# Windowed attention inside a matmul chain: scores of later chunks three slots later, VectorE's work of a round spread, first blocks on 64 keys

## The reference, cut to what matters

```python
# q, k, v: (4, 8, 576, 64); window 64
scores = q @ k.T / 8, masked to 0 <= query - key < 64
attn = softmax(scores); x = (attn @ v) as (2304, 512)
h = ((x @ w1) * (x @ w2)) @ w3 @ w_out          # w1, w2: 512x1024, w3: 1024x1024
h = h @ w_in; g = maximum(0.01 * h, h); out = g @ moe2_w_out   # w_in: 512x2048
```

## Time and profile before

| | before |
|---|---|
| median of 3 runs | 745.69 us |
| profiled execution, its own time | 744.9 us |
| its span | 743.1 us |
| PE busy | 731.5 us (98%) |
| PEld (weight loads) busy | 697.8 us (94%) |
| VectorE (DVE) busy | 533.8 us (72%) |
| ScalarE (ACT) busy | 419.1 us (56%) |
| GpSimd (POOL) busy | 96.7 us (13%) |
| granted TensorE clock | 1.00 of full speed |

### The profile page before, as it was taken

The page is one execution under the profiler, slowest core; times in us unless marked ns, Lnnn a source line. Parts: engine busy times, 40 slices in busy tenths (PEclk is TensorE's granted clock), DMA queues, the critical chain, the costliest instruction groups (busy, mean ns, idle before and its releaser), DMA issues.

```text
span 743.1 us, 13799 instructions
## 1 busy us (share of the span) xinstructions
PE 731.5 (98%) x5032; PEld 697.8 (94%) x5032; DVE 533.8 (72%) x838; ACT 419.1 (56%) x901; POOL 96.7 (13%) x122
## 2 busy tenths in 40 slices
PE   8999899999999999999999999999999999999998
PEld 7778789988889999999999999999999999999998
DVE  6988988788656868788867978658788755454552
ACT  6875587545564345566646656456678544544541
POOL 3433575403343000000000000000000000000000
PEclk9999999999999999999999999999999999999999
DMA  9884577555864289988867988988997457778773
GB/s 340 289 287 140 183 241 214 180 185 154 261 213 146 85 277 335 323 282 315 272 218 265 330 291 278 360 294 281 356 347 287 138 164 235 212 202 242 214 197 120
DMA packets 96835, 181.13 MB, mean 244 GB/s; under 512 B 7936, under 2 KB 55680, under 8 KB 96768
## 3 DMA queue, kind: packets, MB, share of 16 engines
q1 hardware_dynamic: 90032, 166.62, 68.3%
q10 hardware_dynamic: 6736, 13.63, 5.0%
HBM read 111.80 MB, written 68.42 MB: 243 GB/s over the span
## 4 chain that ended last, share of the span: by engine, by line
PE 88%; DVE 4%; DMA 3%; issue 2%; POOL 1%; ACT 1%; SPq 1%; DVEq 0%; ACTq 0%
PE acc L396 16%; PE acc L398 15%; PE acc L397 15%; PE ps_pair L398 5%; PE ps_pair L396 5%; PE ps_pair L397 5%; PE ps_more L396 4%; PE ps_more L398 4%; PE ps_more L397 3%; PE ps_values L398 3%; PE ps_values L396 3%; PE ps_values L397 3%; PE ps_values L1652 2%; PE ps_pair L1674 2%; DMA p_between<-arena 1%
## 5 line engine op out<-in xcount | busy, mean ns | idle before, releaser
L396 PE MATMUL acc<-parts,weights_a 128*128 128x384 f32 (+1 forms) x296 | 104.7, 354 | 1.7 <-DVE arena L1374 0.9
L1443 DVE TENSOR_TENSOR parts<-raw_c,parts 128x768 fp32r<-128x768 f32 x64 | 61.1, 958 | 61.5 <-ACT parts L951 61.4
L398 PE MATMUL acc<-parts,weights_a 128*128 128x384 f32 (+1 forms) x296 | 101.5, 343 | 0.0
L397 PE MATMUL acc<-parts,weights_a 128*128 128x384 f32 (+1 forms) x296 | 101.3, 342 | 0.0
L396 PE MATMUL acc<-parts,weights_b 128*128 128x384 f32 x296 | 100.8, 341 | 0.0
L398 PE MATMUL acc<-parts,weights_b 128*128 128x384 f32 x296 | 99.0, 335 | 0.0
L397 PE MATMUL acc<-parts,weights_b 128*128 128x384 f32 x296 | 99.0, 334 | 0.0
L951 ACT ACTIVATE parts<-raw_c 128x768 fp32r<-128x768 f32 x64 | 54.0, 846 | 69.0 <-DMA raw_c<-g_between 62.9
L396 PEld LDWEIGHTS acc<-parts,weights_a 128*128 128x128 f32 x296 | 55.6, 188 | 6.5 <-issue 2.4
L930 ACT ACTIVATE arena<-arena 128x384 f32<-128x384 f32 x72 | 35.9, 525 | 39.5 <-DVE arena L1316 17.5
L835 ACT ACTIVATE arena<-arena,negmax 128x128 f32<-128x128 f32 x144 | 55.8, 392 | 2.6 <-DVE negmax L1221 2.6
(11 more groups left out here) (215 smaller groups left out, 1840.0 us busy)
## 6 DMA issues: line engine op xcount, KB each, us to landing
g_between<-arena SPq DMA_DIRECT2D x75, 384.0 KB, 4.5
raw_c<-g_between SPq DMA_DIRECT2D x64, 384.0 KB, 3.5
arena<-p_between SPq DMA_DIRECT2D x42, 384.0 KB, 5.1
arena<-qk_steps SPq DMA_DIRECT2D x36, 384.0 KB, 4.1
arena<-v_steps SPq DMA_DIRECT2D x36, 256.0 KB, 3.5
p_between<-arena SPq DMA_DIRECT2D x24, 384.0 KB, 5.3
x_between<-arena ACTq DMA_DIRECT2D x21, 384.0 KB, 5.4
arena<-x_between SPq DMA_DIRECT2D x21, 384.0 KB, 5.5
```

The source lines that it names most:

```text
L396: eng.matmul(out_ap, w_hi, m_hi, start=start, stop=False, skip_group_check=resumed)
L397: eng.matmul(out_ap, w_hi, m_lo, start=False, stop=False, skip_group_check=resumed)
L398: return eng.matmul(out_ap, w_lo, m_hi, start=False, stop=stop, skip_group_check=resumed)
L1443: dve.tensor_tensor(lo, t_source(k), hi.bitcast(F32), ALU.subtract).then_inc(t_lo, 1)
```

## The change

- The scores of chunks 1 and 2 move three slots later (5, 8, ... 38 and 62, 65, ... 95), and with them everything else of a step.
- VectorE's work in a round is put elsewhere: `make_p11` from P2(1) (m = 6) to P3(0) (m = 9); `p_sums` is cut in `p_sum1`, which stays at P4(1), and `p_sums23`, which goes to the next round's P5(0) (m = -1); `make_pt4` goes to the next round's P1(0) (m = 0). `make_p22` now waits for `p_stored[0]` as well.
- At chunk ends `t1` goes from m = 5 to 7, P5's split from 6/7 to 8/9, `t2` from 9 to 10, P2's high part from 8 to 9, P6's high part from 11 to 12.
- First blocks use 64 keys: scores, mask, maximum, exponentials and normalisation have 64 columns per head pair in place of 128. Keys and values of a first block are laid in the first half, and the second half of v's rows is zero. One memset clears that half of `probs[0]` at the start, for step 0.

```diff
-        SCORES[(_c + 1) * CSTEPS + _j] = slot_of(4 * _c, 2 + 3 * _j)
+        SCORES[(_c + 1) * CSTEPS + _j] = slot_of(4 * _c, 5 + 3 * _j)
...
+def width(g):
+    return KW if g % NB else BQ
...
-XS_HI_LAST = {3: P1, 6: P5, 8: P2, 11: P6}
+XS_HI_LAST = {3: P1, 8: P5, 9: P2, 12: P6}
...
-XS_LO_LAST = {4: P1, 5: "t1", 7: P5, 9: "t2", 11: P2}
+XS_LO_LAST = {4: P1, 7: "t1", 9: P5, 10: "t2", 11: P2}
...
+            dve.memset(probs[0][:, :, BQ:KW], 0.0).then_inc(probs_zero, 1)
...
             def make_p22(r):
                 dve.wait_ge(c22_done, 2 * r + 2)
+                if r > 0:
+                    dve.wait_ge(p_stored[0], 16 * r)
...
                 if i == P2:
                     make_c11(r, s)
-                    if s == 1:
-                        make_p11(r)
...
                 if i == P3:
                     make_c12(r, s)
-                    if s == 1:
+                    if s == 0:
+                        make_p11(r)
+                    else:
                         make_p12(r)
                 if i == P4 and s == 1:
                     make_p21(r)
-                    p_sums(r)
-                    make_pt4(r)
+                    p_sum1(r)
+                    if r == AR - 1:
+                        p_sums23(r)
+                        make_pt4(r)
+                if i == P5 and s == 0 and r > 0:
+                    p_sums23(r - 1)
+                if i == P1 and s == 0 and r > 0:
+                    make_pt4(r - 1)
...
-                    last = pe.matmul(ps_scores[x, u], qk[d, g % 2, h // 2 * BQ:(h // 2 + 1) * BQ],
-                                     qk[d, g % 2, QN + u * KW:QN + (u + 1) * KW], start=True, stop=True)
+                    last = pe.matmul(ps_scores[x, u, 0:width(g)], qk[d, g % 2, h // 2 * BQ:(h // 2 + 1) * BQ],
+                                     qk[d, g % 2, QN + u * KW:QN + u * KW + width(g)], start=True, stop=True)
```

More of the change, by code:

```diff
@@ L298, in build @@
         ident_zero = sem("ident_zero")
+        probs_zero = sem("probs_zero")
         ident_made = sem("ident_made")
@@ L763, in normalize @@
                 pool.wait_ge(rsum_done, g + 1)
-                pool.tensor_tensor(probs[g % 3], probs[g % 3],
-                                   rsum[:, r * HP:(r + 1) * HP].unsqueeze(2).to_broadcast([P, HP, KW]),
+                w = width(g)
+                pool.tensor_tensor(probs[g % 3][:, :, 0:w], probs[g % 3][:, :, 0:w],
+                                   rsum[:, r * HP:(r + 1) * HP].unsqueeze(2).to_broadcast([P, HP, w]),
                                    ALU.mult).then_inc(probs_done, 1)
@@ L831, in exps @@
             def exps(g, pairs):
-                r = g % 2
+                r, w = g % 2, width(g)
                 act.wait_ge(max_done, g + 1)
                 for u in pairs:
-                    act.activation(probs[g % 3][:, u], probs[g % 3][:, u], ACT.Exp,
+                    act.activation(probs[g % 3][:, u, 0:w], probs[g % 3][:, u, 0:w], ACT.Exp,
                                    bias=negmax[:, r * HP + u:r * HP + u + 1], scale=1.0,
@@ L1208, in mask_scores @@
             def mask_scores(g):
-                r = g % 2
-                first = g % NB == 0
-                picked = mask_s[:, 1 if first else 0]
+                r, w = g % 2, width(g)
+                picked = mask_s[:, 0 if w == KW else 1, 0:w]
                 dve.wait_ge(scores_done, g + 1)
@@ L1217, in mask_scores @@
                 dve.scalar_tensor_tensor(
-                    out=probs[g % 3], in0=ps_scores, scalar=float(D) ** -0.5, in1=picked.unsqueeze(1).to_broadcast([P, HP, KW]),
+                    out=probs[g % 3][:, :, 0:w], in0=ps_scores[:, :, 0:w], scalar=float(D) ** -0.5,
+                    in1=picked.unsqueeze(1).to_broadcast([P, HP, w]),
                     op0=ALU.mult, op1=ALU.add).then_inc(masked, 1)
                 dve.wait_ge(masked, g + 1)
-                dve.tensor_reduce(negmax[:, r * HP:(r + 1) * HP], probs[g % 3], AX.X, ALU.max,
+                dve.tensor_reduce(negmax[:, r * HP:(r + 1) * HP], probs[g % 3][:, :, 0:w], AX.X, ALU.max,
                                   negate=True).then_inc(max_done, 1)
@@ L1350, in make_p12, with p_sum1 @@
                 dve.tensor_tensor(pa_st[:, 1], u2_sb[:, 0], u2_sb[:, 1], ALU.mult).then_inc(p12_done, 1)
-            def p_sums(r):
+            def p_sum1(r):
                 dve.wait_ge(p11_done, r + 1)
@@ L1360, in p_sums, with p_sums23 @@
                 dve.tensor_tensor(pb_st[:, 0], pa_st[:, 1], pa_st[:, 0], ALU.subtract).then_inc(pt1_made, 1)
+            def p_sums23(r):
                 dve.wait_ge(p22_done, r + 1)
@@ L1656, in turn @@
             def turn(g):
+                if g == 0:
+                    pe.wait_ge(probs_zero, 1)
                 pe.wait_ge(probs_done, g + 1)
@@ L1888 @@
     ks = np.zeros((B, NB, 2, D, HP, 2, BQ), dtype=f)
-    ks[:, :, :, :, :, 1, :] = kt
+    ks[:, 1:, :, :, :, 1, :] = kt[:, 1:]
     ks[:, 1:, :, :, :, 0, :] = kt[:, :-1]
+    ks[:, 0, :, :, :, 0, :] = kt[:, 0]
     qks = np.concatenate([qt.reshape(NSTEP, P, QN), ks.reshape(NSTEP, P, HP * KW)], axis=2)
@@ L1893 @@
     vs = np.zeros((B, NB, 2, BQ, DM), dtype=f)
-    vs[:, :, 1] = vt
+    vs[:, 1:, 1] = vt[:, 1:]
     vs[:, 1:, 0] = vt[:, :-1]
+    vs[:, 0, 0] = vt[:, 0]
     qpos = BQ + np.arange(BQ)[:, None]
@@ L1900 @@
     masks[:, :, 0] = inside
-    masks[:, :, 1, BQ:KW] = inside[:, BQ:KW]
+    masks[:, :, 1, 0:BQ] = inside[:, BQ:KW]
     def pairs(w, nk, nm):
```

## The result

| | before | after |
|---|---|---|
| median of six runs each | 746.0 us (744.01 to 747.83) | 739.92 us (739.72 to 740.43) |
| profiled execution, its own time | 744.9 us | 739.96 us |
| its span | 743.1 us | 738.1 us |

The ratio of the medians is 0.9916 [0.9899, 0.9933]: 6.1 us less. The sign was right, and so were the places in AB from which the forecast took its gain. The size was not: 2.8 us had been forecast, and the profiled executions differ by 5.0, the medians by another 1.1.

The account below looks back on a forecast made before the run. TensorE was taken as the bound, busy 731.5 of 743.1 us. Stalls falling from 7.8 to 5.6 gain 2.2, with restarts and first blocks 2.8: profiled 744.9 to 742.1, median 742.9 us, range 740.3 to 745.3.

Parts of the forecast that it names:

- The waits at 205 and 220: Rounds 5 to 6: two turns waited for late masks, 0.82 and 0.56 us; both waits forecast to go.
- waits did not only move: Rival: GpSimd's work meets the products everywhere, stalls mostly move; gain 0.3 to 2.2 us, about 744.5; chance 0.34.
- the store rival: Chunk ends: `make_p22` meets a store 2 us later, delaying P1(1) and P2(1) by 1.5; 748.9 us; chance 0.04.
- The new stalls, 5.6: Stalls forecast to remain in AB after the change, round 0 and chunk ends, 5.6 us against 7.8 before.
- I take 2.1, nearer the upper end, since rows 5 are this place: Round 0, first turn's wait for its mask: 2.1 us chosen, leaning on trace rows of VectorE's stretched operations there.
- The upper end itself, 2.9: Round 0: first turn 2.9 us late if all VectorE operations are stretched by GpSimd, 1.2 if none.
- The places at the chunk ends: P1(1) and P2(1): 0.8 and 0.2 us in round 4, 0.8 and 0.9 in round 8; chunk 2's first turn 0.8.
- Part 4, "I take 0.4": Four first score blocks with 64 moving columns in place of 128: 0 to 0.9 us saved, 0.4 taken.
- With restarts (0.1 at some): Small extra gain at some vanished stalls, 0.1 us each, added to the 2.2 gained from stalls.
- It lies 0.8 below the median 745.69, so the median goes to 742.9: Last step: the profiled execution's 0.8 us offset carried over, from 742.1 to a median of 742.9.
- VectorE is freed: Rival: round 0's turn waits 1.2 or less, chunk ends cost half; gain 4 to 6.5 us, 740.4; chance 0.18.

Follow-up runs that it names:

- e4: Scores three slots later with the chunk-end splits moved along, VectorE's products and sums as before, against the kernel before: 743.01 us, 0.9956.
- e5: The kernel before, unchanged, profiled once more: 746.53 us at a mean granted clock of 0.998.
- e10: The kernel before with only `make_p11` of round 0 moved from P2(1) to P3(0): 743.77 us, 0.997.
- e1: The kernel before with the first blocks' 64-key form and nothing else: 745.01 us, 0.9984.
- e9: The changed kernel with `make_p12` of round 0 done three times to the same place: 744.31 us, 0.9973 against before.
- e8: The changed kernel with `make_p22` and `make_p12` of round 0 behind the mask of step 14: 739.64 us, 0.9911 against before.

## Why the prediction was wrong

**What held.** The bound, TensorE, and the place and releaser of every stall. Round 0 lost P3's wait and kept one for the mask. The waits at 205 and 220 went, two came in round 8, and `make_p22` met no late store. Both rivals that speak of more waiting fell: waits did not only move (7.8 us became 4.2), and the store rival's condition never came up. e4 shows the other side of it: without the spread, `make_p11` waits for stores 4.6 us.

**Which steps failed.** The sum of the profiled execution was 2.2 us too small (2.8 forecast, 5.0 measured):

- *The new stalls, 5.6.* They measured 4.2. In round 0 "I take 2.1, nearer the upper end, since rows 5 are this place" was the error (1.56). It leaned to all operations stretched, and one of three products met an operation of GpSimd with much left of it; the two low parts kept 0.95, since GpSimd stood idle for 4.06 us before 85.62. The upper end itself, 2.9, doesn't come out of its own terms: 1.2 and three products at 0.48 more are 2.6, and with one stretched low part 3.2. The places at the chunk ends were each about 0.2 too long. Together 1.4.
- *Part 4, "I take 0.4".* It measured 0.8. A score block went from 0.60 to 0.39. That is 0.4.
- *"With restarts (0.1 at some)", 0.2.* Four losses of 0.18 to 0.27 are not there, 0.9. That is 0.7. The 0.4 near 155 and 402 us is hardly the change's: two other profiles, of the kernel before (e5) and of nearly the same (e10), lack most of it.
- Against that, this execution's first product matmul starts 0.4 later. It did so at 5.01 to 6.01 in the other profiles, with the memset and without, so nothing shows it to be an effect of the change. About 0.1 I can't place.

**The step that no sum could mend** is the last: "It lies 0.8 below the median 745.69, so the median goes to 742.9". The offset was carried over as if it were a constant of the measurement. It was not. The profiled execution of before ran at full clock, as 18 of 57 later runs did (0.999 or 1.000); the others were slower, by 2.3 us in the median beside e1 to e4, and e5 shows 1.4 us of this behind round 0's two gaps. The change takes one of the two gaps away, none of its six runs has a lower clock, and its median is the profiled execution's own time (739.92 and 739.96). The offset went from about 1 us to none. Three experiments bear on it: e5 has the stretch at half clock, e9 brings it on with a longer gap, and in e10 the runs with a lower clock are gone when one product moves. The six runs of before in the first table have no clock on record, and only one execution of before was seen with the stretch, so that round 0 is the place in the others too is argued from e10 and not seen.

The measured time lies near the rival "VectorE is freed", whose condition on round 0, a wait of 1.2 or less, did not come true (1.56). That its number came near is partly luck: a part of the gain came by the clock, which it doesn't speak of.

## What to carry to other kernels

A wait of TensorE can cost more than its idle time when it stands near another. Here 0.4 us less idle time in round 0 came with 2.6 us less in the median (interval 1.2 to 3.3). So, before carrying a profiled execution's offset over, compare its mean granted clock with that of the other runs, and if it differs look in the windows behind the largest gaps. Match the same matmuls in two traces before giving a price to a stretch or a gap. And of a change with three parts, run each alone: here one part made the shift needless, and one piece of it helped in one round of twelve and hurt at the chunk ends.

## What the runs showed of the chip that I had not expected

- Idle times of 0.80 and 1.31 us within about 3 us of a nearly full stream of matmuls were followed by 3.4 us at the 1.2 GHz level in one profiled execution and by none in another, with the same two gaps to 0.01 us. Of 57 runs 39 have a mean clock of 0.997 or 0.998.
- A VectorE product and a GpSimd operation that read SBUF delay whichever starts second, by what is left of the first less about 0.15 us: 0.48 us lost by the product at 86.04 (0.62 left), and 0.34 by the weight sum at 88.66 (0.50 left).
- Sixteen 64-row matmuls with 64 moving columns take 0.39 us where those with 128 take 0.60, with the stationary operand unchanged.
- In the first 10 us an execution can have its matmuls nearly twice as far apart (0.43 against 0.23 for 512 columns) while the view shows a granted clock of 1.00: 2.5 us later in AB in the profile of e8, 0.9 in that of e10, not counted in the mean clock.
